# First group of a fused attention and feed-forward kernel: queries of its first head pair loaded first, one order for all its head pairs, shorter idle products

## The reference

```python
# q, k, v: (4 batches, 8 heads, 576 tokens, 64), float32
kv = einsum('bhsd,bhse->bhde', k, v)            # no softmax
out = einsum('bhsd,bhde->bhse', q, kv)
out = out / sqrt(mean(out * out, -1) + 1e-6) * g_norm
x = out.transpose(0, 2, 1, 3).reshape(2304, 512)
h = x @ w_in                                    # 512 -> 2048
x = (h * sigmoid(h)) @ w_out                    # 2048 -> 512
y = ((x @ w_a) * (x @ w_b)) @ w_out2            # 512 -> 1536 -> 512
```

## Time and profile before

| | |
|---|---|
| median of 3 runs | 872.4 us (872.25 to 872.96) |
| the profiled execution | 873.04 us, its span 871.2 us |
| PE busy | 860.4 us, 99% of the span |
| first idle product / `kv` of pair 0 / first `q_kv` | 1.56 / 6.98 / 11.25 us |
| `kv` of pairs 1, 2, 3 | 13.37 / 21.38 / 31.76 us |
| first product of the feed-forward layer (L794) | 38.49 us |

### The profile page before, as it was taken

One profiled execution on the slowest core, in us unless ns is written; L12 is line 12 of the kernel. 1 busy time (PEld: TensorE's weight loads), 2 busy tenths in 40 slices (PEclk: granted clock), 3 DMA queues, 4 the chain that ended last, 5 costly groups with the idle time before them and its releaser, 6 DMA issues.

```text
span 871.2 us, 16097 instructions
## 1 busy us (share of the span) xinstructions
PE 860.4 (99%) x6208; PEld 813.8 (93%) x6208; DVE 510.6 (59%) x776; ACT 279.0 (32%) x465; POOL 610.1 (70%) x889
## 2 busy tenths in 40 slices
PE   8899999999999999999999999999999999999998
PEld 5699999999999999999999999999999999999997
DVE  4665656757886666665765355364484553544636
ACT  3764434534543323222532122121242211212210
POOL 2566545666578777766778697797889876877760
PEclk9999999999999999999999999999999999999999
DMA  9664123111011111111101111021011330210104
GB/s 300 158 156 106 49 57 75 50 49 49 26 49 49 46 28 50 50 49 49 49 25 49 50 49 49 25 63 60 25 49 49 109 98 25 74 49 25 49 25 109
DMA packets 47002, 55.56 MB, mean 64 GB/s; under 512 B 11728, under 2 KB 32464, under 8 KB 46928
## 3 DMA queue, kind: packets, MB, share of 16 engines
q1 hardware_dynamic: 44192, 49.55, 19.9%
q10 hardware_dynamic: 2736, 4.98, 1.8%
HBM read 49.81 MB, written 4.72 MB: 63 GB/s over the span
## 4 chain that ended last, share of the span: by engine, by line
PE 98%; DVE 1%; issue 1%; ACT 0%; POOL 0%; POOLq 0%
PE ps L777 49%; PE ps L863 8%; PE ps L864 8%; PE ps L865 8%; PE ps L885 6%; PE ps L887 6%; PE ps L886 6%; PE ps L794 3%; PE ps L737 2%; PE ps L747 1%; PE ps L989 1%; PE ps L709 1%; PE ps L723 1%; DVE o_sb L1350 0%; DVE stat L1331 0%
## 5 line engine op out<-in xcount | busy, mean ns | idle before, releaser
L777 PE MATMUL ps<-x_hi,w_hi 128*128 128x288 f32 x1064 | 229.8, 297 | 0.5 <-issue 0.3
L777 PE MATMUL ps<-x_lo,w_hi 128*128 128x288 f32 x1064 | 228.1, 296 | 0.0
L777 PE MATMUL ps<-x_hi,w_lo 128*128 128x288 f32 x1064 | 226.8, 295 | 0.0
L777 PEld LDWEIGHTS ps<-x_hi,w_hi 128*128 128x128 f32 x1064 | 179.0, 188 | 13.7 <-issue 5.1
L777 PEld LDWEIGHTS ps<-x_hi,w_lo 128*128 128x128 f32 x1064 | 171.7, 189 | 0.0
L777 PEld LDWEIGHTS ps<-x_lo,w_hi 128*128 128x128 f32 x1064 | 169.9, 188 | 0.0
L1142 ACT COPY kept<-ps 128x576 f32<-128x576 f32 x114 | 73.2, 642 | 288.1 <-PE ps L777 287.6
L523 POOL TENSOR_SCALAR w_hi<-wt 128x256 fp32r<-128x256 f32 x152 | 69.9, 460 | 123.4 <-PE ps L777 116.4
L1473 DVE TENSOR_TENSOR xy<-xy,ps 128x384 f32<-128x384 f32 (+1 forms) x188 | 94.0, 510 | 89.0 <-PE ps L865 88.7
L863 PE MATMUL ps<-g_hi,d_hi 128*128 128x384 f32 x384 | 129.0, 336 | 0.2
L864 PE MATMUL ps<-g_lo,d_hi 128*128 128x384 f32 x384 | 128.9, 336 | 0.0
(11 more groups left out here) (111 smaller groups left out, 1236.7 us busy)
## 6 DMA issues: line engine op xcount, KB each, us to landing
raw<-in_moe_w_out_dram SPq DMA_DIRECT2D x28, 512.0 KB, 3.6
raw<-in_moe_w_in_dram SPq DMA_DIRECT2D x15, 512.0 KB, 3.5
raw<-in_moe_w_a_dram SPq DMA_DIRECT2D x12, 512.0 KB, 3.5
raw<-in_moe_w_b_dram SPq DMA_DIRECT2D x12, 512.0 KB, 3.5
kvq<-in_k_dram SPq DMA_DIRECT2D x8, 576.0 KB, 5.5
out_dram<-xy SPq DMA_DIRECT2D x26, 128.0 KB, 2.4
kvq<-in_v_dram ACTq DMA_DIRECT2D x4, 576.0 KB, 11.4
kvq<-in_v_dram SPq DMA_DIRECT2D x4, 576.0 KB, 5.9
```

The costliest lines, as they stand in the source:

```text
L777: mm = pe.matmul(ps[:, bank + s, 0:PART], w, x[:, n, c, s * PART:(s + 1) * PART], start=(begins and first), stop=last, skip_group_check=no ...
```

## The change

The first head pair's queries are issued ahead of its keys and values on both queues. On PE the three `q_turn` units of pair 0 stand ahead of its `kv`. Pair 0 takes the order of the others. The idle products use the identity as both operands, on 128 columns instead of 512, eight ahead of the transposes and six behind them; the zeros and their wait are gone. DVE takes up the turned queries of pair 0 before the keys-times-values.

```diff
-    WARM = (3, 2)
+    WARM = (8, 6)
...
+            sp.dma_start(*queries(0, 0)).then_inc(q_in[0], 16)
             for h in range(PAIRS):
                 sp.dma_start(*heads(0, h, 0)).then_inc(kv_in[h], 16)
-                sp.dma_start(*queries(h, 0)).then_inc(q_in[h], 16)
+                if h:
+                    sp.dma_start(*queries(h, 0)).then_inc(q_in[h], 16)
...
-                    zeros = wt[:, 0:2, :].rearrange("p a n -> p (a n)")
-                    pe.matmul(ps[:, first_bank(1, 0), :], ident[:], zeros, start=True, stop=True)
+                    pe.matmul(ps[:, BANK_D, 0:P], ident[:], ident[:], start=True, stop=True)
...
-            pe.wait_ge(cleared, 1)
             warm(WARM[0])
-            kv(0, 0)
-            warm(WARM[1])
             for j in range(JS):
                 q_turn(0, 0, j, first_bank(0, j))
+            warm(WARM[1])
+            kv(0, 0)
             for h in range(PAIRS):
                 for j in range(JS):
-                    if h > 1:
+                    if h:
                         o_turn(0, h - 1, j, result_bank(h - 1, j))
                     q_kv(0, h, j, prod_bank(h, j))
                 if h + 1 < PAIRS:
                     kv(0, h + 1)
                     for j in range(JS):
-                        if h == 0:
-                            o_turn(0, 0, j, result_bank(0, j))
                         q_turn(0, h + 1, j, first_bank(h + 1, j))
...
+            nc.scalar.dma_start(*queries(0, 1)).then_inc(q_in[0], 16)
             for h in range(PAIRS):
                 nc.scalar.dma_start(*heads(0, h, 1)).then_inc(kv_in[h], 16)
-                nc.scalar.dma_start(*queries(h, 1)).then_inc(q_in[h], 16)
+                if h:
+                    nc.scalar.dma_start(*queries(h, 1)).then_inc(q_in[h], 16)
...
-            nc.vector.memset(wt[:, 0:2, :], 0.0).then_inc(cleared, 1)
             nc.vector.memset(kv_sb[:], 0.0).then_inc(cleared, 1)
...
-            second_kv_keep()
             for j in range(JS):
                 qT_keep(0, 0, j, first_bank(0, j))
+            second_kv_keep()
             for h in range(PAIRS):
...
                 for j in range(JS):
                     normalise(0, h, j)
-                    if 0 < h < PAIRS - 1:
+                    if h < PAIRS - 1:
                         qT_keep(0, h + 1, j, first_bank(h + 1, j))
```

More of the change, by code:

```diff
@@ L1069, in kv_keep @@
                     act.wait_ge(o_mm, JS * (n - 1))
-                act.wait_ge(cleared, 2)
+                act.wait_ge(cleared, 1)
                 for odd, bank in enumerate((BANK_D, BANK_D + 1)):
@@ L1287, in _ @@
                     kv_keep(0, h + 1)
-                if h == 0:
-                    for j in range(JS):
-                        keep(0, 0, j, result_bank(0, j))
                 if h in (1, 2):
@@ L1316, in _ @@
         def _(dve):
-            nc.vector.memset(wt[:, 0:2, :], 0.0).then_inc(cleared, 1)
             nc.vector.memset(kv_sb[:], 0.0).then_inc(cleared, 1)
-            dve.wait_ge(cleared, 2)
+            dve.wait_ge(cleared, 1)
             def qT_keep(G, h, j, bank):
@@ L1689, in _ @@
                     normalise(0, h, j)
-                    if 0 < h < PAIRS - 1:
+                    if h < PAIRS - 1:
                         qT_keep(0, h + 1, j, first_bank(h + 1, j))
-                if h == 0:
-                    for j in range(JS):
-                        qT_keep(0, 1, j, first_bank(1, j))
             first_pair()
```

## The result

The changed kernel takes 876.2 us, the kernel before 871.75 us (medians of 18 runs each in the same sessions). The ratio is 1.0053, with a 95% interval of 1.0042 to 1.0064: 3.7 to 5.6 us slower. I had forecast 871.2 us and a range of 868.6 to 873.9. The profiled execution of the changed kernel took 877.13 us, with a span of 875.3 against 871.2 before. A profile shows one execution, and both lie high: the one before (873.04) 1.3 us above its kernel's median, that of the changed kernel 0.9 above.

What follows compares the result with a forecast made beforehand. PE's late instruction blocks during the input loads were taken to bound the stage before the feed-forward layer. Its start moves from 38.49 to 37.4, 1.1 us, plus 0.1 for the sequencer: 872.4 - 1.2 = 871.2 us, range 868.6 to 873.9.

Steps and rivals of the forecast that it cites:

- The blocks: PE's instructions are fetched in blocks of 256, one per 7.9 us while the 16 DMA engines are full of input loads.
- the three new places of the pauses: With 36 instructions more ahead, every block begins or ends 36 instructions earlier in PE's program.
- the order of pair 0 is hidden: Pair 1 is done 1.5 us later, at 23.0, yet kv of pair 2 still ends 1.6 before the block of 25.85.
- the cost of a low clock behind a long pause is covered by the next pause: If the clock falls in pair 1's long pause, 1 to 1.5 us more are covered by the pause of 1.6.
- keys and values land when the queries did: 9.0. ... Pairs 1 to 3 have the same bytes before them and land as before.: Reordered input loads: pair 0's keys and values land at 9.0 (8.5 to 9.4), later pairs at 13.65, 20.41 and 26.72.
- The queries themselves, put at 5.2: Pair 0's queries, loaded first, land at about 5.2 us, with the load running at 400 GB/s from 3 us.
- At 9.0 + 1.28 x 116/144 = 10.05: The first block begins 28 instructions before the end of pair 0's kv, at 10.05 instead of 11.3, 1.2 us earlier.
- rival C: Clock low until after 10: first block at 11.4, pair 1's loss of 1.5 not paid back, 874.1 us; chance 0.18.
- The later ones follow at 7.95 and 7.85: The next two blocks come at 18.0 and 25.85, inside q_turn of pair 1 and at the head of pair 2's.
- I take it that the new one fits in: The fourth block, requested at 25.85 in a DMA gap, arrives by 30, so pair 3's kv goes through: 0 cost.
- D: The DMA gap is missed: fourth block at 33.7, feed-forward layer 0.2 later than before, 872.6 us; chance 0.14.
- Rival B: Block fetches don't bind, PE's pauses are data waits or packets come sooner: 866.7 us, partly 869.9; chance 0.18.

Runs made afterwards that it cites:

- a_order_before: The changed kernel with pair 0's own old order put back on PE, ACT and DVE: 876.91 us, ratio 1.0061 to the kernel before.
- b_order_after: The kernel before with the one order of head pairs alone: 871.8 us, ratio 1.0002.
- a_long_warm: The changed kernel with three idle products of 512 columns ahead of the transposes, one of 512 and two of 128 behind, on zeros: 874.97 us, ratio 1.0044.
- a_queries_act: The changed kernel with both halves of pair 0's queries issued first by ACT, SP beginning with the keys: 878.93 us, ratio 1.0096.
- b_plus36: The kernel before with its three first idle products of 512 columns cut into twelve of 128, 36 instructions more: 873.03 us, ratio 1.0011.
- a_minus36: The changed kernel with its short idle products merged into as many columns of long ones, 36 instructions fewer: 875.25 us, ratio 1.0036.
- b_hold: The kernel before with loads of pairs 2 and 3 held back until keys and values of the pair before had landed: 870.53 us, ratio 0.9996.
- b_rest: The kernel before with the short idle products and one order of pairs, loads and pair 0's kv first as before: 869.6 us, ratio 0.9981.

## Why the prediction was wrong

**What held.** That the stage ahead of 38.5 us counts one for one. The blocks, with their size, and the three new places of the pauses. That the order of pair 0 is hidden (a_order_before, b_order_after). That queries-first makes `kv` the late one. That the cost of a low clock behind a long pause is covered by the next pause. It was forecast for pair 1 and came at pair 2, which took 6.17 us from its first transposes to the end of its products, where pair 3 took 4.83; PE stood for the next block anyway.

**The step that failed first: "keys and values land when the queries did: 9.0. ... Pairs 1 to 3 have the same bytes before them and land as before."** Values landed at 7.6, keys at 10.6; pair 1's queries at 17.5, not 13.65. The same bytes in another order moved at 250 instead of 300 GB/s over the first 15 us. The queries themselves, put at 5.2, were there for POOL at 6.24: the three us from 3 to 6 moved 316, 230 and 224 GB/s and not 400. (The "241 GB/s over the 2 us before" is the stretch from 2 to 4 us; from 1 to 3 us it was 50.) My range of 8.5 to 9.4 for the landing allowed for transfers not draining alike, but was made from the rows of transfers in the old order, and treated a queue as a pipe of fixed rate.

**Then the start of the first block.** "At 9.0 + 1.28 x 116/144 = 10.05": it began at about 11.95. PE was also held at the low clock (0.50 from 8.0 to 11.4 us), as rival C has it, but a_long_warm shows that the keys would have held `kv` until 10.5 anyway. Of the 1.85 us late at `kv`, about 1.5 are the keys and 0.3 the clock and what follows from it. So C's late start came, but mostly by another cause than C's. On the clock: it rose at 4.6 us and fell at 8.0, after a stretch in which PE idled from 5.0 to 6.8 and then turned queries. The row neither proves nor refutes the rule of the Trainium skill that I weighed ("TensorE: Matmul & The Clock Gate", section "Part 4: PE-mode transpose"), that transposes don't count as PE being busy in the same way.

**The intervals.** "The later ones follow at 7.95 and 7.85": 7.7, 9.3 and 8.5. Three equal numbers from one execution looked like a constant; they are a waiting time. The packets moved 4.9, 6.7 and 6.0 us after the block before had begun, against 5.3, 5.1 and 4.9 in the kernel before. The longest interval that ended in a pause for issue is 9.3 us, in three of the 16 profiles (the changed kernel, a_order_before, a_queries_act).

**The fourth block.** "I take it that the new one fits in": into the gap between the two loads, so that PE would not stop for it. It did stop, until 37.4, inside `kv` of pair 3. Rivals C and D had this step. The 1.6 us that lie behind it because of its place were not in the sum. But the gap was not missed by coming late. The gap moved along with the loads, and the block before began at 28.89, at its start (each row ends with the clock, the DMA share and the GB/s):

```profile
28.00:30.00 2.00, 1.11 (x6) 1.11 (x6) 0.27 (x1) 0.00 (x0) 0.00 (x0) 0.62 0.60 127
30.00:32.00 2.00, 2.00 (x14) 1.67 (x14) 2.00 (x5) 0.35 (x1) 1.65 (x4) 0.53 0.29 44
```

From 29.2 to 31.2 us the DMA engines had next to nothing to do, and still the packet moved only at 34.9, when group 1's loads filled them again. The two packets after it, where loads are few, moved within 2 us of a block's begin in every trace. So for this block the rule that a request goes out with the block's begin and waits behind queued packets is not enough, and what held it is open.

**The rivals and the range.** C had everything that came: the late first block, the order of pair 1 not paid back, the fourth block in `kv` of pair 3. It was too small twice: the first block began at 11.95 and not 11.4, and the three intervals add up to 25.45 us and not 23.7. That gives 2.3 us, from its 40.2 to 42.5 for the start of the layer. No rival had slower loads or longer intervals, and the top of the range, 873.9, lay under C's own 874.1. The forecast was a gain of 1.2 us, and the loss is 4.5 by the medians; the two are 5.65 us apart. That forecast and measurement differ by 5.0 only is luck: the three runs that the forecast started from lay 0.65 high (872.4 against 871.75).

**Rival B** (the fetches don't bind) is refuted by b_plus36, a_minus36 and b_hold. The rule of the Trainium skill, "Runtime: NRT & Kernel Launch", section "Instruction fetch mechanics", that the fetch of a block is mostly hidden, holds here behind the input loads: no pause for issue over 0.3 us after 45 us, in the kernel before and in the changed one. While they run it doesn't, by pauses of up to 3.4 us in the changed kernel; in b_rest, by 0.4 us.

## What to carry to other kernels

If PE pauses for "issue" inside a run of equal instructions, count the instructions between the ends of such pauses; if the counts are equal, the program itself is late, and bulk loads queued early are the first suspect: here, holding them back brought the first blocks earlier. Then every instruction added ahead shifts where all later blocks end, so two edits that cost or do nothing alone can gain together, and each must be timed with the others in. Before a load is moved ahead of another, look at what the first needed transfer was worth on time: here it was the keys, and no order in which `kv` of the first pair began after 10 us came within 2 us of the old one.

## What the runs showed that I had not expected

- Loads that begin with the 64-partition halves of the queries on both queues move at 249 to 251 GB/s over the first 15 us in five kernels, those that begin with the 128-partition keys and values at 278 to 300. Both kinds have packets of the same size. Why is open: putting the queues in step did nothing, and moving the queries to one queue tested something else.
- Two queues with equal bytes ahead don't land together: values at 7.6, keys at 10.6 us in the changed kernel.
- A profile can put a wait for a block down to another engine: at 19.27 in the kernel before (DVE) and at 23.43 in b_rest (in part; POOL). The count of instructions tells.
- The spread of a kernel's runs depends on the kernel: the 18 runs of the changed kernel lie between 873.6 and 880.1 us, the 11 of b_rest, in another session, between 868.9 and 871.2.
